# Attention units taken in threes, with a third buffer of biased scores and another order of early loads and stores

## What is computed

```python
B, H, S, D = 2, 8, 768, 64
scores = q @ k.T / 8 - slope[h] * dist          # only keys 0..7 and the last 96 keys are kept
a = exp(scores - max(scores)); a = a / (sum(a) + 1e-9)
x = (a @ v) -> [B, S, 512]
theta = x @ w_theta                              # first layer
zr, zi = x * cos(theta), x * sin(theta)
u = x + w_tok_r @ zr + w_tok_i @ zi
x = u + relu(u @ w_ch)
h = relu(x @ w_in)                               # second layer, d_ff = 1024
out = (h * sigmoid(conv3(h))) @ w_out
```

## Time and profile before

| what | value |
|---|---|
| median of 3 runs | 394.95 us (394.83 to 395.25) |
| the profiled execution | 394.86 us, of it span of instructions 393.1 us |
| PE busy in the span | 385.1 us (98%) |
| DVE, ACT, POOL busy | 251.8, 223.7, 139.9 us |
| attention on PE | from 6.64 to 90.48 us of the span |
| the granted clock of TensorE | 1.00, its full 2.4 GHz |

### The profile page before, as it was taken

How to read it: one execution, slowest core, us unless ns; L and a number is a source line. 1 busy time by engine, 2 the same in 40 slices (tenths; PEclk the granted TensorE clock), 3 DMA queues, 4 the chain that set the end, 5 groups by cost and what they waited for, 6 DMA issues and landing times.

```text
span 393.1 us, 6248 instructions
## 1 busy us (share of the span) xinstructions
PE 385.1 (98%) x2214; PEld 337.7 (86%) x2214; DVE 251.8 (64%) x633; ACT 223.7 (57%) x441; POOL 139.9 (36%) x119
## 2 busy tenths in 40 slices
PE   7999999999999999999999999999999999999996
PEld 3888889888788888888898899998999899899985
DVE  5977777765787899998998744665553343443410
ACT  3777777774776785424544352855863644644531
POOL 2079999992345200400000072033852232232230
PEclk9999999999999999999999999999999999999999
DMA  7998879244000362412312430003300200200022
GB/s 230 419 410 351 291 286 368 115 198 88 0 0 3 107 242 80 161 48 74 82 40 69 159 107 0 3 1 117 98 3 0 80 2 1 80 2 0 2 80 80
DMA packets 15728, 43.98 MB, mean 112 GB/s; under 512 B 4560, under 2 KB 4816, under 8 KB 15696
## 3 DMA queue, kind: packets, MB, share of 16 engines
q1 hardware_dynamic: 15696, 43.57, 31.3%
HBM read 32.16 MB, written 11.40 MB: 111 GB/s over the span
## 4 chain that ended last, share of the span: by engine, by line
PE 91%; ACT 4%; DVE 2%; issue 1%; DMA 1%; ACTq 0%
PE bank L514 29%; PE bank L666 19%; PE bank L723 17%; PE bank L561 9%; PE bank L546 6%; PE bank L533 5%; PE bank L646 3%; PE bank L626 1%; PE bank L572 1%; PE bank L679 1%; ACT h_sb L998 1%; DMA woutraw<-w_out_in 1%; ACT pr L796 1%; DVE bank L1454 0%; ACT bank L1006 0%
## 5 line engine op out<-in xcount | busy, mean ns | idle before, releaser
L666 PE MATMUL bank<-b_ops,a_ops 128*128 128x512 f32 x324 | 75.5, 391 | 0.0
L514 PE MATMUL bank<-vT,win 128*128 128x386 f32 x384 | 73.3, 340 | 0.9 <-ACT h_sb L998 0.9
L514 PEld LDWEIGHTS bank<-vT,win 128*128 128x128 f32 x384 | 68.3, 188 | 3.4 <-issue 1.0
L666 PEld LDWEIGHTS bank<-b_ops,a_ops 128*128 128x128 f32 x324 | 60.5, 188 | 12.3
L723 PE MATMUL bank<-wout,g 128*128 128x512 f32 x288 | 69.5, 390 | 0.0
L488 POOL TENSOR_TENSOR g<-gf,g 128x384 fp32r<-128x384 f32 x32 | 32.6, 1019 | 94.2 <-ACT g L1018 94.2
L723 PEld LDWEIGHTS bank<-wout,g 128*128 128x128 f32 x288 | 53.9, 188 | 9.7
L1454 DVE SCALAR_TENSOR_TENSOR bank<-h_sb,convw,bank 128x384 f32<-128x384 f32 x32 | 19.9, 622 | 65.9 <-ACT bank L1006 65.9
L998 ACT ACTIVATE h_sb<-bank 128x386 f32<-128x386 f32 x32 | 15.8, 494 | 51.8 <-PE bank L514 48.6
L796 ACT ACTIVATE pr<-biased,small 128x232 f32<-128x232 f32 (+1 forms) x96 | 39.6, 464 | 1.3 <-DVE small L1126 1.3
L807 ACT ACTIVATE pT<-bank 128x512 f32<-128x512 f32 (+1 forms) x48 | 26.9, 561 | 19.8 <-PE bank L561 18.1
(11 more groups left out here) (98 smaller groups left out, 572.8 us busy)
## 6 DMA issues: line engine op xcount, KB each, us to landing
qk_sb<-qk_laid SPq DMA_DIRECT2D x7, 792.0 KB, 9.4
v_sb<-v_laid SPq DMA_DIRECT2D x6, 780.0 KB, 8.7
w_raw<-w_tok_laid SPq DMA_DIRECT2D x6, 768.0 KB, 13.7
a_kept<-stage SPq DMA_DIRECT2D x6, 768.0 KB, 4.0
a_ops<-a_kept SPq DMA_DIRECT2D x6, 768.0 KB, 4.9
a_kept<-stage SPq DMA_DIRECT2D x9, 384.0 KB, 2.8
a_ops<-a_kept SPq DMA_DIRECT2D x9, 384.0 KB, 3.1
out<-ob SPq DMA_DIRECT2D x12, 256.0 KB, 2.1
```

Source lines behind the costliest of these rows:

```text
L514: last = pe.matmul(dst, w[a], m[b], start=(i == 0 and j == 0), stop=(i == n - 1 and j == 2))
L666: last = pe.matmul(y_bank(s)[:], a_ops[:, slot, hi, blk, :], b_ops[:, side, blk, lo, :], start=(blk == 0 and j == 0), stop=(blk == NT - 1 ...
```

## The change

- The attention is issued in batches of three units. `scores(k)` makes units 3k to 3k+2, and NK = 16. The PE loop has 16 turns, each with three times transposes and weighted V; the two tiles of x come behind the loop.
- `biased` has a third buffer, `biased_third`, at 179.125 KB in SBUF; `small` has three places. `maxima(u)` waits for the exponentials of u - 3 in place of u - 2. The orders of `copy_p` and `exps` on ACT, and the numbers of buffers of `pr`, `pT`, of the transposes' banks and of the output banks, are as before.
- `s_bank(u)`: units 0 and 1 of a batch share banks 0 and 1 (one half each), the third has banks 2 and 3, its half changing from batch to batch. Ahead of the first unit of a batch PE waits for the maxima up to unit u - 2, ahead of the third for those up to u - 3. `scores_ready` rises by 2 behind the second unit and by 1 behind the third.
- DVE takes maxima three units ahead and puts one unit's quotient between each two. `make_bias` still makes two heads at the end of each turn, which is now three units long.
- SP: `w_raw(0)` is loaded ahead of the third pair's q, k and v; later loads and stores stand in another order. The four stage buffers change places, so that `turns(0)` waits for 13 staged parts and the stores of buffers 0 and 3 only; `high_z(0)` waits for those of 1 and 2.

The core of the diff:

```diff
-    NK = NU // 2
+    NK = NU // 3
-        small = att("small", [P, 2, 8], F32)
+        small = att("small", [P, 3, 8], F32)
+        biased_third = at("biased_third", [P, 2, BAND], F32, 179.125)
+        biased_of = [biased[:, 0], biased[:, 1], biased_third[:]]
-        stage = [at("stage%d" % n, [P, 2, SB], F32R, kb) for n, kb in enumerate((161, 167, 182, 188))]
+        stage = [at("stage%d" % n, [P, 2, SB], F32R, kb) for n, kb in enumerate((182, 161, 167, 188))]
+        def s_bank(u):
+            side, half = (0, u % 3) if u % 3 < 2 else (1, u // 3 % 2)
+            return psum[:, 2 * side:2 * side + 2, 256 * half:256 * half + 256]
...
             def scores(k):
+                for u in range(3 * k, 3 * k + 3):
+                    p, i = divmod(u, NT)
...
+                    if k and u % 3 == 0:
+                        pe.wait_ge(max_ready, 2 * (u - 1))
+                    if k and u % 3 == 2:
+                        pe.wait_ge(max_ready, 2 * (u - 2))
...
-                last.then_inc(scores_ready, 2)
+                    if u % 3:
+                        last.then_inc(scores_ready, 3 - u % 3)
...
-                for k in range(NK + 1):
+                for k in range(NK):
                     if k + 1 < NK:
                         scores(k + 1)
+                    for u in range(3 * k, 3 * k + 3):
+                        transpose_p(u)
                         if u >= 2:
                             weighted_v(u - 2)
+                for t in range(2):
+                    x_tile(t)
+                    weighted_v(NU - 2 + t)
...
-                    act.wait_ge(staged, NA)
-                    for m in range(4):
+                    act.wait_ge(staged, NA - 2)
+                    for m in (0, 3):
                         act.wait_ge(stored_a[m], 16 * ((NA + 3 - m) // 4))
...
-                dve.wait_ge(scores_ready, 2 * (u // 2) + 2)
+                dve.wait_ge(scores_ready, max(u, u // 3 * 3 + 1) + 1)
-                if u >= 2:
-                    dve.wait_ge(probs_ready, u - 1)
+                if u >= 3:
+                    dve.wait_ge(probs_ready, u - 2)
...
+                for k in range(NK):
+                    for u in range(3 * k, 3 * k + 3):
+                        if u + 3 < NU:
+                            maxima(u + 3)
+                        if u >= 2:
+                            normalize(u - 2)
                     for h in (2 * k + 2, 2 * k + 3):
```

More of the change, by code:

```diff
@@ L281, in banded, with store @@
             def banded():
[L282 to L286, removed]
-                        store_a(m)
-                        if m == 4:
-                            load_w_raw(2)
-                    kept += count
+                def store(first, last):
+                    for m in range(first, last):
+                        store_a(m)
+                load_qk(3)
+                load_v(3)
+                load_qk(4)
+                load_v(4)
+                load_qk(5)
+                store(0, 5)
+                load_w_raw(2)
+                load_v(5)
+                load_qk(6)
+                store(5, 6)
+                load_v(6)
+                load_qk(7)
+                store(6, 10)
+                load_v(7)
+                store(10, NA)
             def general():
@@ L313, in _ @@
             load_v(1)
+            load_w_raw(0)
             load_qk(2)
             load_v(2)
[L316 removed]
             load_w_raw(1)
@@ L518, in scores @@
             def scores(k):
[L519 to L528, removed]
+                for u in range(3 * k, 3 * k + 3):
+                    p, i = divmod(u, NT)
+                    if u == 0:
+                        pe.wait_ge(qk_first, 32)
+                    if i == (0 if p else 2):
+                        pe.wait_ge(qk_in[p % 3], qk_landed(p))
+                    if k and u % 3 == 0:
+                        pe.wait_ge(max_ready, 2 * (u - 1))
+                    if k and u % 3 == 2:
+                        pe.wait_ge(max_ready, 2 * (u - 2))
                     cols = slice(0, BAND) if i else slice(OWN, BAND)
@@ L532, in scores @@
                         rows = slice(h * D, (h + 1) * D)
-                        last = pe.matmul(S_BANK[u % 4][:, h, cols], qk_sb[rows, p % 3, i * P:(i + 1) * P],
+                        last = pe.matmul(s_bank(u)[:, h, cols], qk_sb[rows, p % 3, i * P:(i + 1) * P],
                                          qk_sb[rows, p % 3, S + c0:S + c1], start=True, stop=True)
-                last.then_inc(scores_ready, 2)
+                    if u % 3:
+                        last.then_inc(scores_ready, 3 - u % 3)
             def transpose_p(u):
@@ L795, in exps @@
                     act.wait_ge(max_ready, 2 * u + h + 1)
-                    last = act.activation(pr[:, u % 4, h, cols], biased[:, u % 2, h, cols], ACT.Exp,
-                                          bias=small[:, u % 2, 2 + h:3 + h], scale=-1.0)
+                    last = act.activation(pr[:, u % 4, h, cols], biased_of[u % 3][:, h, cols], ACT.Exp,
+                                          bias=small[:, u % 3, 2 + h:3 + h], scale=-1.0)
                 last.then_inc(probs_ready, 1)
@@ L866, in high_z @@
                 act.wait_ge(zf_ready, n + 1)
+                if n == 0:
+                    for m in (1, 2):
+                        act.wait_ge(stored_a[m], 16 * ((NA + 3 - m) // 4))
                 act.activation(b_ops[:, 1, n, 0, :], zr[0][:, n, :], ACT.Copy).then_inc(z_hi, 1)
@@ L1173, in banded, with normalize @@
                 maxima(1)
-                for k in range(NK + 1):
-                    if k + 1 < NK:
-                        maxima(2 * k + 2)
-                        maxima(2 * k + 3)
-                    if k == NK:
-                        low_x(0)
-                    for u in (2 * k - 2, 2 * k - 1):
-                        if u >= 0:
-                            denominators(u)
-                            reciprocals(u)
-                            divide(u)
+                maxima(2)
+                def normalize(u):
+                    denominators(u)
+                    reciprocals(u)
+                    divide(u)
+                for k in range(NK):
[4 more added lines that the diff above has]
+                            normalize(u - 2)
                     for h in (2 * k + 2, 2 * k + 3):
```

21 lines of the change are left out of this document (9 added, 12 removed).

## The result

| | us | runs |
|---|---|---|
| before, median | 395.05 (394.83 to 395.47) | 6 |
| after, median | 398.88 (398.39 to 399.51) | 6 |
| ratio | 1.0096, 95% interval 1.0085 to 1.0107 | |
| span of the profiled execution, before and after | 393.1 and 397.3 | |

The changed kernel is slower by 3.8 us. The forecast was 398.6, its range 396.4 to 400.0. In all runs reported here the granted clock is 0.998 to 1.000 on average, but for two runs of `fours_exps_ahead` further down (0.987 at 398.0 us, 0.983 at 400.6 us), of which there is no trace.

The account below looks back on a forecast made before the run. PE's own pace was taken to set the attention. Start +2.06, steady part +1.9 and end -0.1 gave +3.86, by kinds +3.7; 394.9 + 3.7 = 398.6 us, 8 in 10 within 396.4 to 400.0.

Parts of the forecast that it names:

- The batches: Batches of scores on PE: 24 become 16, each switch costing 0.34 us, so 2.7 us less.
- The loop of ACT and PE: Copy, exps, transposes need 1.78 us against PE's 1.40: PE loses 0.43 at units 3k + 2, 0.22 behind a tile 0.
- The start: From the beginning to unit 6's transposes on PE: at 19.82 us against 17.76, +2.06.
- The steady part: Six pairs of heads in mid-attention: 10.57 us a pair against 10.26, +1.9 in all.
- The end: From unit 42's first transposes to theta: 11.1 us against 11.18, -0.1, with waits at units 45 and 47.
- The sum: Whole attention: 2.06 + 1.9 - 0.1 = +3.86 us, or +3.7 counted by kinds; +3.7 was taken.
- What was costed at nothing: Third biased buffer costed at 0, as PE had no idle time from that wait; moved loads and stores cost nothing.
- POOL: POOL starts 3.3 us later, near 25.2, and stops at some 93.7; covered by 4.5 us before turns(0).
- (a): Rival, batches win: no wait at 3k + 2 because the copy is early; 392.9 us, chance 0.09.
- (b): Rival, half: waits about half as long or a cheaper start; +0.3 to +2.2, 396.4 us, chance 0.09.
- (c): Rival, the clock: PE's stands at the start drop it to 1.2 GHz; at most +4, 402 us, chance 0.04.
- (d): Rival, POOL too late: the stored part holds up turns(0); +1 to +2 on top, 400 us, chance 0.05.

Follow-up runs that it names:

- fours_exps_ahead: Changed kernel with units in batches of four, exps one unit further ahead on ACT, scores(1) and some of DVE's biases moved: 394.12 us, ratio 0.9983.
- twos_exps_ahead: Kernel before, in batches of two, with only exps on ACT put one unit further ahead: 394.51 us, ratio 0.9989.
- threes_exps_ahead: Changed kernel with only exps on ACT put one unit further ahead of the copy, buffers and waits kept: 392.55 us, ratio 0.9942.
- twos_all_else: Kernel before, in batches of two, with the change's third biased buffer, stage places, weaker turns(0) wait and load and store order: 394.93 us, ratio 1.0002.
- threes_act_more: Changed kernel with an unused 128x4 copy added on ACT behind each copy_p: 399.91 us, ratio 1.0122 to the kernel before.
- after_again: Changed kernel run once more, nothing changed, to check its late first scores: 398.96 us, ratio 1.0096 to the kernel before.
- fours_loads: fours_exps_ahead with only SP's order of early loads changed, q, k and v of the first three pairs first: 391.63 us, ratio 0.9915.

## Why the prediction was right, step by step

- **The batches.** Eight fewer at 0.34 was 2.7. Measured 0.32 each (`twos_exps_ahead` against `threes_exps_ahead`), 2.5.
- **The loop of ACT and PE.** The wait at 3k + 2 was put at 0.38 + 0.05 and measured at 0.38 + 0.05. Behind a tile 0 it was put at 0.17 + 0.05 and is 0.18 in all: 0.16 in the wait (1.45 from 21.57 to 23.02, against 1.29 in `threes_exps_ahead`) and 0.02 in what follows up to unit 9. The one bare instance in the earlier trace rows gave the length for all of them.
- **The start.** 19.82 - 6.64 = 13.18 from the first scores to unit 6 was worked out, 20.46 - 7.29 = 13.17 measured; each step on the way agrees within 0.02 (unit 0 3.51 and 3.52, unit 2 5.18 and 5.18, unit 3 7.37 and 7.37, unit 5 10.38 and 10.36). Against before it costs 2.05.
- **The steady part.** Six pairs 63.31 (20.46 to 83.77) against 61.54 in the earlier trace rows: +1.77, put at +1.9. A pair is 10.55, put at 10.57. Two terms are mis-sized, and they cancel in part: the wait behind a tile 0 with its restart, 0.18 for 0.22, and the batch, 0.32 for 0.34.
- **The end.** 94.70 - 83.77 = 10.93 against 11.18: -0.25, put at -0.1. The waits at units 45 and 47 were 0.61 and 0.38, put at 0.7 and 0.4.
- **The sum.** 2.05 + 1.77 - 0.25 = 3.57, put at 3.7 to 3.86. The medians differ by 3.83. No trace shows where the 0.26 above 3.57 lie; the one thing that moved beside the attention in the traces is the start of the scores (7.29 and 7.08 for 6.64), which the prediction did not have. So it is in part luck that 398.6 lies within 0.3 of 398.88: the sum took the attention 0.1 to 0.3 too dear, and the late start made up for it.
- **What was costed at nothing.** The third buffer, the stage places and the loads are worth 0 in twos (`twos_all_else`); threes with two buffers of biased scores were not tried. Here the rule of the Trainium skill, Perfetto Trace Analysis, section Optimization Strategy, that a repeating gap on the engine which should be full can mean too few buffers, did not fit the buffer that was added, and did fit the one that was not: with a third `pT` the gap went and 5.7 us with it. The same was had with no buffer, by the order on ACT, and 0.7 more.
- **POOL.** First sum at 26.08, which less the 0.65 is 25.4, put at 25.2; it ends at 94.39, put at 93.7 (and 0.65). Covered, as said.
- **Rivals.** (a) fell with the gaps in the middle, (b) with their length. (c), the clock, did not come: in stretches of 5 us the granted clock is 1.00 all through the attention. The prediction put the first stand of PE there at 0.5 (8.3 to 8.8), though its own sum had 0.82; it was 0.86, and the second 0.79. (d) did not come in after; where `th_k` does wait for a store, in four of the other kernels, it costs nothing.

## What to carry to other kernels

Before work is regrouped to save switches on the full engine, look for what the mixed order covered: find each loop between two engines that goes through few buffers, take its bare length from the one place in the trace where nothing lies between (here 1.78 us against 1.40 of PE's own), and count for the new order how often nothing lies between. If the loop is longer, loosen it first, by another order on the helping engine or another buffer: the same regrouping cost 3.8 us without that (395.05 to 398.88) and won 2.0 with it (394.51 to 392.55). Then ask of the loads which of them the larger group now wants sooner.

## What the runs showed of the hardware that was not expected

The same instructions ahead of the first scores took different times. Four products of 128x512 in bf16 lead up to them; in after:

```profile
5.67 1.69 PE L642 MATMUL bank<-idle 128*128 128x512 bf16 x4 [0.54 <-issue]
```

and in `threes_act_more`, with the same instructions there:

```profile
5.64 1.03 PE L643 MATMUL bank<-idle 128*128 128x512 bf16 x4 [0.72 <-issue]
6.60 1.28 PE L549 MATMUL bank<-qk_sb 64*128 64x128 f32 x12
```

From their start to the first scores it is 1.62 in after (0.41 a product), 1.47 in `after_again`, 1.35 in `fours_loads`, 1.04 in before, and 0.96 here (0.24 a product). The granted clock is shown as 1.00, the 2.4 GHz level, in all of them over this stretch. The longest and the shortest lie nearly a factor of two apart, as the two levels do, but the record shows no fall, so the cause is not shown. All that follows in an execution moves by up to 0.8 us (scores from 6.53 in `threes_exps_ahead` to 7.29). Whether it depends on the kernel or on chance is open: after and `after_again` are both late, `threes_act_more`, which has the same start, is early.

A small ACT operation of 128x4 has a busy time of 0.20 and delays the next by 0.09 to 0.10. Costs of short operations in a chain are better read from start to start, and from operations of the same kind: the exponentials' steps pointed to 0.2, the copies' to 0.06.
